# A new order of transfers at the start of a bucketed attention kernel: SyncE's queue, two transfers from GpSimd, and small VectorE operations moved

## The reference

```python
q_bits = (einsum('bhsd,dk->bhsk', q, proj) > 0)      # 6 bits: a bucket from 0 to 63
k_bits = (einsum('bhsd,dk->bhsk', k, proj) > 0)
mask = q_bucket[:, :, :, None] == k_bucket[:, :, None, :]
scores = where(mask, scale * q @ k.T, -1e9)
attn = exp(scores - max); attn = attn / (sum + 1e-9)
x = (attn @ v)                                       # 16 heads of 768 x 64 -> 1536 x 512
e_idx = argmax(x @ w_gate)                           # one of 8 experts a row
y = gate_w * sigmoid(x @ w_output_gate)[e_idx] * (relu(x @ w1[e]) @ w2[e])
out = elu(y @ w_in) @ w_out
```

## Time and profile before

| | |
|---|---|
| median of 3 runs | 769.79 us (769.7 to 772.74) |
| profiled execution | 770.78 us, its span 768.8 us |
| busy, share of the span | PE 98%, weight load of PE 82%, DVE 55%, POOL 48%, ACT 45% |
| granted PE clock, mean | 0.998 of full speed |

### The profile page before, as it was taken

The page is one execution under the profiler, slowest core; times in us unless marked ns, Lnnn a source line. Parts: engine busy times, 40 slices in busy tenths (PEclk is TensorE's granted clock), DMA queues, the critical chain, the costliest instruction groups (busy, mean ns, idle before and its releaser), DMA issues.

```text
span 768.8 us, 12446 instructions
## 1 busy us (share of the span) xinstructions
PE 755.6 (98%) x4247; PEld 631.0 (82%) x4247; DVE 425.7 (55%) x844; ACT 345.5 (45%) x656; POOL 367.5 (48%) x251
## 2 busy tenths in 40 slices
PE   8999999999999999999999999999999999999996
PEld 6677777777776788888888888898899889989985
DVE  8887777777665644454544444588147216414610
ACT  7766667777764214432343210175046117404710
POOL 5666567878820799777977870234200120010001
PEclk9999999999999999999999999999999999999999
DMA  5423424113111777655775620530100010000000
GB/s 142 106 66 90 121 76 111 51 49 88 27 46 26 276 244 257 196 192 166 232 226 172 227 75 28 176 113 0 50 34 1 28 55 1 1 28 14 0 15 27
DMA packets 42763, 73.67 MB, mean 96 GB/s; under 512 B 20336, under 2 KB 24080, under 8 KB 42704
## 3 DMA queue, kind: packets, MB, share of 16 engines
q1 hardware_dynamic: 29680, 30.07, 13.3%
q10 hardware_dynamic: 9584, 31.53, 12.5%
q0 software_dynamic: 3440, 11.28, 4.5%
HBM read 60.48 MB, written 11.28 MB: 93 GB/s over the span
## 4 chain that ended last, share of the span: by engine, by line
PE 61%; issue 29%; DVE 3%; POOL 2%; ACT 2%; DMA 1%; SPq 0%; POOLq 0%; DVEq 0%
PE pair_s L1450 14%; PE pair_t L1465 14%; PE pair_u L1259 8%; PE bank_b L1274 8%; PE pair_s L1246 5%; PE pair_t L1246 4%; PE pair_u L1425 2%; PE bank_b L1296 1%; POOL out L625 1%; PE pair_s L1503 1%; DVE g_lo L1189 1%; PE bank_a L1216 1%; DVE exps L891 1%; POOL y_raw L619 1%; POOL w_part L501 1%
## 5 line engine op out<-in xcount | busy, mean ns | idle before, releaser
L501 POOL TENSOR_TENSOR w_part<-w_raw,w_part 128x1024 fp32r<-128x1024 f32 x80 | 190.2, 2404 | 57.3 <-ACT w_part L735 57.2
L735 ACT ACTIVATE w_part<-w_raw 128x1024 fp32r<-128x1024 f32 x72 | 73.8, 1054 | 126.8 <-PE pair_t L1465 84.9
L1552 PE MATMUL pair_t<-w_part,g_hi 128*128 128x512 f32 x384 | 118.9, 391 | 0.3 <-POOL w_part L501 0.3
L625 POOL DMA_INDIRECT out<-o_sb,token x12 | 11.7, 978 | 208.5 <-DVE o_sb L1159 208.5
L1450 PE MATMUL pair_s<-w_part,xs_t 128*128 x456 | 108.8, 394 | 0.2 <-issue 0.2
L1465 PE MATMUL pair_t<-w_part,hid_t 128*128 x456 | 109.0, 394 | 0.0
L1450 PEld LDWEIGHTS pair_s<-w_part,xs_t 128*128 128x128 f32 x456 | 84.3, 188 | 17.7 <-issue 0.9
L1465 PEld LDWEIGHTS pair_t<-w_part,hid_t 128*128 128x128 f32 x456 | 84.4, 189 | 16.8
L677 ACT ACTIVATE exps<-exps,nmax 128x768 f32<-128x768 f32 x96 | 88.5, 926 | 1.7 <-DVE exps L891 1.7
L834 ACT ACTIVATE elu<-elu 128x384 f32<-128x384 f32 x64 | 33.6, 525 | 122.8 <-DVE elu L1179 122.7
L1259 PEld LDWEIGHTS pair_u<-first,exps 128*128 128x128 f32 x564 | 64.2, 140 | 24.3 <-issue 16.3
(11 more groups left out here) (218 smaller groups left out, 1092.8 us busy)
## 6 DMA issues: line engine op xcount, KB each, us to landing
w_raw<-in_moe_w ACTq DMA_DIRECT2D x48, 512.0 KB
w_raw<-in_moe_w SPq DMA_DIRECT2D x16, 512.0 KB
ys_sorted<-ys SPq DMA_DIRECT2D x19, 256.5 KB, 3.6
w_raw<-in_moe_w_in ACTq DMA_DIRECT2D x8, 512.0 KB
raw<-in_q SPq DMA_DIRECT2D x16, 192.0 KB, 3.4
raw<-in_k SPq DMA_DIRECT2D x16, 192.0 KB, 3.5
v_nat<-in_v SPq DMA_DIRECT2D x16, 192.0 KB, 2.6
x_rows<-rows_sb SPq DMA_DIRECT2D x32, 96.0 KB, 2.6
```

The lines of the kernel that those rows point to most:

```text
L501: pool.tensor_tensor(chunk_of(w_part, n, 1, c), w_raw[n % 2][c][:, :], chunk_of(w_part, n, 0, c).bitcast(F32), ALU.subtract).then_inc(s_wl ...
L735: act.activation(chunk_of(w_part, n, 0, c), w_raw[n % 2][c][:, :], ACT.Copy).then_inc(s_whi, 1)
L1552: mm = pe.matmul(pair_t[:, t % 2, :], gp[:, f, j * P:(j + 1) * P], w_out_p[:, wp, f, :], start=f == 0 and m == 0, stop=f == FT - 1 and m == 2)
```

## The change

Five edits, all of them about what comes before what:

- SyncE: v of head 0 goes out at head 2, rows of bits and v of head 1 at head 3, both as before; from head 4 on q and k of head g go out first and the rows of bits and v of head g - 2 behind them. The constants go out behind the loads of head 3 and not of head 2.
- Two of head 1's four `k_a` rows are issued by GpSimd, ahead of its work on head 1, with a semaphore of their own, `s_soft`.
- GpSimd's copies into `last_e` and `last_w` come behind head 2 and not behind head 1.
- VectorE: the two `minus_w` copies come right behind `sign(0)`.
- VectorE: `inverse` comes in the third group of a head and not in the second.

```diff
@@ SyncE
             def place_bits(g):
                 sp.wait_ge(s_sgn, g + 1)
-                for i in range(4):
+                for i in range(POOL_ROWS if g == 1 else 0, 4):
...
             def load_head(g):
-                if g >= 3:
-                    place_bits(g - 2)
+                if g == 2:
+                    load_v(0)
+                if g == 3:
+                    place_bits(1)
+                    load_v(1)
                 if g >= 2:
-                    load_v(g - 2)
                     sp.wait_ge(s_bits, g - 1)
...
                 load_qk(g, 0)
                 load_qk(g, 1)
+                if g >= 4:
+                    place_bits(g - 2)
+                    load_v(g - 2)
                 if g >= 6:
                     store_rows(g - 6)
...
                 load_head(g)
-                if g == 2:
+                if g == 3:
                     sp.dma_start(cst[:, P:], const[:, P:]).then_inc(s_cst, 16)
-                if g == 3:
                     load_gates()
@@ GpSimd
             pool.wait_ge(s_cp, prepared(0))
+            pool.wait_ge(s_sgn, 2)
+            for i in range(POOL_ROWS):
+                pool.dma_start(k_a[D:KEYED, 1, i * QUART:(i + 1) * QUART].bitcast(F32),
+                               bit_k[i * BIT_K + BIT_ROWS:i * BIT_K + 2 * BIT_ROWS, :].bitcast(F32)).then_inc(s_soft, 16)
...
-                if g == 1:
+                if g == 2:
                     pool.wait_ge(s_cst, 16)
@@ VectorE
             sign(0)
+            dve.tensor_scalar(minus_w[0:D, :], proj_w[0:D, :], 1.0, None, ALU.mult).then_inc(s_minus, 1)
+            dve.tensor_scalar(minus_w[D:P, :], proj_w[D:P, :], -1.0, None, ALU.mult).then_inc(s_minus, 1)
             mask_even(0)
...
             least(1)
-            dve.tensor_scalar(minus_w[0:D, :], proj_w[0:D, :], 1.0, None, ALU.mult).then_inc(s_minus, 1)
-            dve.tensor_scalar(minus_w[D:P, :], proj_w[D:P, :], -1.0, None, ALU.mult).then_inc(s_minus, 1)
             least(2)
...
-                if part == 1 and g >= 2:
+                if part == 2 and g >= 2:
                     inverse(g - 2)
```

More of the change, by code:

```diff
@@ L77 @@
 KEYED = 64 + BIT_ROWS
+POOL_ROWS = 2
 BT = 3
@@ L303, in program @@
         s_mask = sem("s_mask")
+        s_soft = sem("s_soft")
         s_minus = sem("s_minus")
@@ L395, in program @@
         prepared = lambda g: COPIES * g + 1
+        masked = lambda g: 16 * (8 * g - POOL_ROWS)
         rounded_q = lambda g: 2 * g - 1 if g >= 3 else g + 2
@@ L658, in big_bits @@
                 if g >= 2:
-                    act.wait_ge(s_mask, 128 * (g - 1))
+                    act.wait_ge(s_mask, masked(g - 1))
                 act.activation(bit_q[:, :], bit_k[:, :].bitcast(F32), ACT.Copy, scale=-BIG).then_inc(s_big, 1)
@@ L900, in sign @@
                     if g >= 2:
-                        dve.wait_ge(s_mask, 128 * (g - 1))
+                        dve.wait_ge(s_mask, masked(g - 1))
+                        dve.wait_ge(s_soft, 16 * POOL_ROWS)
                         dve.wait_ge(s_big, g - 1)
@@ L1234, in scores @@
                 else:
-                    pe.wait_ge(s_mask, 128 * g)
+                    pe.wait_ge(s_mask, masked(g))
+                    pe.wait_ge(s_soft, 16 * POOL_ROWS)
                 if g == 0:
```

## The result

The changed kernel takes 772.74 us (median of 21 runs, 770.04 to 775.36) against 769.27 us (21 runs) before: ratio 1.0043, 95% interval 1.0032 to 1.0054. By that ratio it is slower by 3.3 us; the medians are 3.5 us apart. The forecast was 771.0 us in a range of 768.3 to 773.2 us. Its direction and place were right; the size was not: +1.2 us was forecast.

What follows compares the result with a forecast made beforehand. PE was taken to bound attention after 34 us, with holes only in the start-up. Head 2's mask, wanted at 34.27 us, would come at 17.6 + 17.83 = 35.4 us: 769.79 + 1.2 = 771.0 us, range 768.3 to 773.2 us.

Steps and rivals of the forecast that it cites:

- minus_w: VectorE start-up: first copy blocked by GpSimd until 8.15 us, so `sign(1)` ends at 9.95 us instead of 8.73 us.
- GpSimd's issues: Ahead of GpSimd's work on head 1: two transfers at 1.0 us each, 2.0 us; head 1 prepared at 17.6 us.
- SyncE's order: SyncE's start-up queue: 17.83 us from head 1 prepared to head 2's mask, including 1.21 us for head 4's q and k.
- What the wait costs: PE ahead of head 2's scores: mask at 35.4 us against 34.27 us, costing +1.2 us.
- Later heads: Heads 3 to 15: new order taken as zero; PE has 1.05 us of idle time in 184.90 us to give.
- The constants: GpSimd's copies one head later: head 3 prepared some 3 us later, about 36 us, needed near 48 us, so hidden.
- inverse: VectorE: moving it removes the 1.69 us block at 28.65 us; at most 1.7 us of VectorE come back.
- Head 1's hole: PE ahead of head 1's first scores: with fewer SyncE rows, most of the 1.29 us hole goes.
- rival A: Start-up: head 2's mask isn't late, 767.1 to 769.8 us; chance 0.28.
- B: Start-up: GpSimd's two issues are dear, 775.0 us at 3 us each; chance 0.05 over 3.85 us, 0.09 between +2.4 and +3.85.
- my own mechanism: Start-up: head 2's mask late by 0.4 to 2.4 us, giving 770.2 to 772.2 us; chance 0.55.
- C: Every head: the change of order makes each head's mask slide, if its preparation ended after its sign; chance 0.03.

Runs made afterwards that it cites:

- e12: The kernel before with the two `minus_w` copies right behind `sign(0)`, nothing else: 769.56 us, ratio 1.0001.
- e11: e8 with all rows of head 1 issued by SyncE, none by GpSimd: 769.26 us, ratio 1.0003 to the kernel before.
- e5: The changed kernel with the two `minus_w` copies back between `least(1)` and `least(2)`: 770.41 us, ratio 1.0023 to the kernel before.
- e4: The changed kernel with `cst` and GpSimd's copies of constants at their old places: 770.95 us, ratio 1.0015 to the kernel before.
- e7: The changed kernel with the edits of e2 and e4 together: 769.00 us, ratio 0.9990 to the kernel before.
- e8: e7 with the two `minus_w` copies moved behind `least(5)`: 768.08 us, ratio 0.9982 to the kernel before.
- e9: The kernel before with two of head 1's `k_a` rows issued by GpSimd, nothing else: 770.10 us, ratio 1.0003.
- e1: The changed kernel with 26 small added matmuls on PE ahead of head 2's first scores: 771.42 us, ratio 1.0019 to the kernel before.
- e6: The changed kernel with all four `k_a` rows of head 1 issued by SyncE: 772.68 us, ratio 1.0045 to the kernel before, six runs.
- e2: The changed kernel with head 2's rows of bits issued ahead of q and k of head 4: 769.64 us, ratio 1.0000 to the kernel before.
- e3: The kernel before with q and k ahead of the rows of bits and v from head 5 on: 768.92 us, ratio 0.9990.
- e10: The kernel before with `inverse` in the third group of a head, nothing else: 769.66 us, ratio 1.0002.

## Why the prediction was right or wrong

**`minus_w`: right.** Forecast: blocked to 8.15 us, `sign(1)` at 9.95 us; measured 8.13 and 9.96 us, and e12 has the same 1.38 us copy. The other side shows in e11, beside an idle GpSimd: 0.17 and 0.18 us.

**GpSimd's issues: right in sum, by luck.** 2.0 us were taken for two issues of 1.0 us each; from the end of `sign(1)` to L537 it took 1.98 us, but 0.66 us of it before the first issue, for which I had no term, and only 1.27 us for both. That is half a gather each. The transfers landed 1.7 us after their issue. The Trainium skill, "DMA: Bandwidth & Descriptors", section "Anatomy of one DMA — SWDGE (gpsimd) path", gives about 2.0 us for a small one. The trace has a little less here (2.3 us in e5), and more where the load of `cst` (660 KB) goes out just ahead of them: 3.9 us in e4 and e7, 4.3 us in e8, 4.8 us in e9. The warning of the Trainium skill that I weighed in the prediction ("SBUF — State Buffer", section "SBUF: two separate sides": VectorE's two-port operations keep GpSimd from writing its descriptors) could not be seen here: no copy of that kind ran beside the issues. L888, which has two SBUF inputs, ran from 9.88 to 10.82 us, beside the start of the first issue; it does so in e5, e7 and e8 as well, where the two issues take the same 1.27 us, so no run shows them without it.

**SyncE's order: the place right, one term mis-sized.** q of head 3 went out at 17.57 us (forecast 17.6), and the terms behind it were 1.21, 0.62, 6.60 and 0.73 us as forecast. The term "newly ahead of the rows of bits, q and k of head 4, 1.21 us" measured 2.41 us, since the issue of k alone took 1.85 us. The rest agrees too: 5.41 us to the issue of the last row (5.42 us forecast) and 1.94 us from there to the scores (2.1 us forecast). The mask was 2.2 us late and not 1.2 us. In e1, e4, e5 and e6 the same issue took 1.17, 0.60, 0.60 and 0.60 us: such long issues come and go, also with other transfers (the k load of the kernel before, 1.02 us), and what makes them is open. e2 shows that this order is what costs. How often the issue is long in runs without a profile isn't known.

**What the wait costs: the step that failed.** "PE asked for this mask at 34.27 us. It now gets it at 35.4 us: +1.2 us" counted the wait at its own length alone. With 2.70 us of idle time the clock fell, and that cost 2.75 us more in the profiled execution. e1 shows it apart: the same late mask with PE at work has the clock at 1.00 and 2.5 us less span. The three executions that kept the clock without such help (770.04 to 771.62 us) lie about the forecast of 771.0 us, the other 18 above it. The rows that spoke for no loss were those of the kernel before, where 1.29 us of idle time left the clock at 1.00; I did not ask what a longer one does.

**Later heads: taken as zero, in fact -1.05 us in the profile.** I said of the 1.05 us that PE had them to give, and did not look at what they were. The new order takes the stores from behind q and k (e3), and every kernel with this order is without the hole. The medians of e3 are too close to those before to show the gain.

**The constants: I took them as hidden; they were only covered.** GpSimd's copies push the scaling of head 3's k back, and VectorE waits 2.67 us for it at 26.7 us. In the changed kernel the late mask covers this; e4 without the copies has PE done with `project(3)` at 32.9 us and not at 33.8 us. That a later wait hides this delay is luck, not slack.

**`inverse`: a gain under the mask's cover,** as forecast. Alone (e10) it brings PE to head 2 0.9 us earlier in the profile and shows no gain in the median.

**Head 1's hole: a premise that was wrong.** I read the 1.29 us ahead of head 1 as the price of SyncE's queue, to be won back by two rows fewer. e3, e10 and e12 issue the same rows from SyncE and don't have it (see e3). This changed nothing in the sum, as I counted no gain from it, but rival A's best time of 767.1 us rests on it in part.

Of the rivals, A did not come: the block was there. B's mechanism (dear issues on GpSimd) is refuted by 1.27 us for two, though the time came out close to its bound of 3.85 us, by the clock and one long issue. The measured time lies above the 770.2 to 772.2 us that I gave to my own mechanism; it lies within the range only because the range had room for dear GpSimd issues, and that is luck. C is refuted: the later heads gained.

## What to carry to other kernels

A wait of PE is not priced by its length alone: some of 1.41 to 2.70 us here took the clock with them and cost 1.6 to 2.75 us more. Where a wait can't be avoided, cheap matmuls inside it are worth trying. One profile is one execution: look at the clocks and times of the others before taking its account for the median, and look for a hole in a second profile before planning to fill it. When a load is moved ahead of small transfers on a full queue, count from the earliest wait that opens the queue to the last small transfer, for the first heads on their own; an order that is free in the steady state (e3) can be the whole loss in the start-up (e2). Before calling a hole of 1 us in the steady state noise, look which instruction stands ahead of it: here it was a store behind two loads.

## What the runs showed of the hardware

- The clock and idle time of PE, ahead of head 2: 0.37, 0.40, 0.55, 0.75, 1.31 and 1.49 us left it at 2.4 GHz (e12, e7, e2, e5, e3, e6), 1.41, 1.52, 1.67 and 2.70 us did not (e11, e4, e9, the changed kernel). 1.41 us fell and 1.49 us did not, so the length of this wait alone doesn't decide.
- What the fall cost: the work of 4.36 us took 5.93 to 5.96 us in e4, e9 and e11, where the clock was back by 38 us, and 7.11 us in the changed kernel, where it was back after 42 us.
- It falls in some executions of the kernel before as well. Of the 35 timed beside e1 to e4, 32 have a mean clock of 0.998 or more and take at most 770.65 us; the other three have 0.993 to 0.997 and take 771.78 to 774.08 us.
- A 64x32 copy of VectorE takes 0.17 to 0.19 us with no GpSimd instruction beside it. Behind one over 64x768 it ends 0.03 to 0.04 us after that instruction: 1.41 us in the changed kernel, 1.72 us in e5.
- Two small transfers cost GpSimd 0.66 us of start and 1.27 us for both (the start in the changed kernel, e5, e7 and e8, the issues in all eight kernels that have them); SyncE needs 1.49 us (`q_a`, 2.98 / 2) to 1.7 us (`k_a`) for two.
- PE starts 1.22 or 1.23 us after SyncE has issued the last row of head 2's mask where it waits for it, in eight kernels; in e6 it was 1.91 us. In two executions one share of the mask came 2.07 us (before, head 1) and 1.64 us (e3, head 2) behind the others.
